# One fused kernel of attention, expert layer and rational layer, all three stages written anew

## What is computed

```python
# attention: B, H, S, D = 2, 8, 768, 64; block 32, window 16
k_sum = k.reshape(B, H, nb, block, D).max(axis=3)
v_sum = v.reshape(B, H, nb, block, D).mean(axis=3)
scores_l = scale * np.matmul(q, k.transpose(0, 1, 3, 2))      # |i - j| < window only
scores_s = scale * np.einsum('bhsd,bhnd->bhsn', q, k_sum) + np.log(block)
a = softmax(concat(masked scores_l, scores_s)); out = a @ concat(v, v_sum)
# expert layer: 1536 tokens x 512, 8 experts of 512 x 1024 x 512, one expert for each token
logits = xn @ en.T / tau; expert_idx = np.argmax(logits, axis=1)
out[mask] = gate_w[mask, None] * (np.maximum(x[mask] @ w1[e], 0.0) @ w2[e])
# rational layer: 512 -> 2048 -> 512
h = x @ w_in; P = a[0] + a[1]*h + a[2]*h*h + a[3]*h*h*h
Q = 1.0 + abs(b[0]) * abs(h) + abs(b[1]) * h*h
out = (P / (Q + 1e-06)) @ w_out
```

## Time and profile before

| | |
|---|---|
| runs | 886.36, 894.67, 916.50 us; median 894.67 |
| profiled execution: span from first to last instruction | 909.4 us |
| instructions | 13113 |
| PE busy, PEld busy | 776.2 us (85%), 641.1 us (71%) |
| DVE, ACT, POOL busy | 505.2, 410.6, 92.5 us |
| mean granted TensorE clock | 0.860 |
| DMA | 80.45 MB, 66388 packets, 43568 of them under 512 B |

### The profile page before, as it was taken

How to read it: one execution, slowest core, us unless ns; L and a number is a source line. 1 busy time by engine, 2 the same in 40 slices (tenths; PEclk the granted TensorE clock), 3 DMA queues, 4 the chain that set the end, 5 groups by cost and what they waited for, 6 DMA issues and landing times.

```text
span 909.4 us, 13113 instructions
## 1 busy us (share of the span) xinstructions
PE 776.2 (85%) x3557; PEld 641.1 (71%) x3558; DVE 505.2 (56%) x911; ACT 410.6 (45%) x752; POOL 92.5 (10%) x107
## 2 busy tenths in 40 slices
PE   2369999999992198887998998849999989999995
PEld 2268989999992176666876876727778768787884
DVE  4822333335455044655333133148999899989996
ACT  2122222234442153655334244146666666666663
POOL 1120302111002300000000000050000000000000
PEclk9655555569995599999999999968999999999999
DMA  9332131133230454787126125030000100000001
GB/s 209 125 107 58 43 99 43 51 95 92 79 107 35 173 210 172 280 279 271 46 92 254 46 74 180 24 92 12 25 21 3 47 0 0 0 25 22 1 0 47
DMA packets 66388, 80.45 MB, mean 88 GB/s; under 512 B 43568, under 2 KB 43568, under 8 KB 65464
## 3 DMA queue, kind: packets, MB, share of 16 engines
q1 hardware_dynamic: 57224, 54.39, 19.5%
q0 software_dynamic: 6048, 20.45, 6.6%
q10 hardware_dynamic: 3088, 5.26, 1.6%
HBM read 63.48 MB, written 16.61 MB: 88 GB/s over the span
## 4 chain that ended last, share of the span: by engine, by line
PE 54%; DVE 18%; DMA 9%; ACT 8%; issue 5%; SPq 3%; POOL 1%; ACTq 0%; DVEq 0%; POOLq 0%
PE bank L1122 12%; PE bank L949 8%; DMA xg<-x_by_slot 7%; PE bank L1101 6%; PE bank L1009 5%; PE bank L1034 5%; PE bank L1175 5%; PE bank L1190 5%; PE bank L1032 4%; PE bank L1007 3%; DVE qd L905 3%; DVE pb L907 3%; DVE rr L906 3%; ACT rr L604 2%; DVE qd L898 2%
## 5 line engine op out<-in xcount | busy, mean ns | idle before, releaser
L1190 PE MATMUL bank<-weights,G 128*128 128x512 f32 x576 | 144.4, 400 | 6.1 <-DVE G L830 5.9
L1175 PE MATMUL bank<-X2T,weights 128*128 (+1 forms) x576 | 145.8, 403 | 1.6 <-DVE X2T L830 1.6
L1190 PEld LDWEIGHTS bank<-weights,G 128*128 128x128 f32 x576 | 108.9, 190 | 34.2 <-DVE G L830 5.8
L1175 PEld LDWEIGHTS bank<-X2T,weights 128*128 128x128 f32 x576 | 109.9, 192 | 28.6 <-issue 2.4
L1101 PE MATMUL bank<-weights,XT 128*128 (+1 forms) x456 | 116.8, 406 | 5.7 <-DVE XT L830 5.7
L1122 PE MATMUL bank<-weights,HT 128*128 x456 | 118.6, 419 | 2.4 <-DVE HT L830 2.4
L488 ACT ACTIVATE es<-es,nmx 128x182 f32<-128x182 f32 x96 | 42.8, 446 | 146.6 <-DVE nmx L736 146.5
L1122 PEld LDWEIGHTS bank<-weights,HT 128*128 128x128 f32 x456 | 90.0, 200 | 23.9 <-issue 2.6
L1101 PEld LDWEIGHTS bank<-weights,XT 128*128 128x128 f32 x456 | 85.2, 191 | 28.2 <-issue 9.6
L736 DVE CUSTOM_DVE_ANT_0 es<-bank,mask_now 128x182 f32<-128x182 f32 x96 | 33.2, 348 | 127.5 <-PE bank L1009 109.7
L830 DVE TENSOR_TENSOR HT<-bank,HT 128x512 fp32r<-128x512 f32 x38 | 24.5, 686 | 97.3 <-ACT HT L549 97.3
(11 more groups left out here) (167 smaller groups left out, 1188.3 us busy)
## 6 DMA issues: line engine op xcount, KB each, us to landing
raw_early<-in_moe_w_dram SPq DMA_DIRECT2D x14, 1024.0 KB, 5.4
raw_late<-in_moe_w_dram SPq DMA_DIRECT2D x14, 1024.0 KB, 8.8
x_by_slot<-x_all ACTq DMA_DIRECT2D x5, 1024.0 KB, 4.4
xg<-x_by_slot POOLq DMA_DIRECT2D x19, 256.0 KB, 5.5
y_by_slot<-yo POOLq DMA_DIRECT2D x19, 256.0 KB, 2.4
raw_early<-in_moe_w_dram POOLq DMA_DIRECT2D x4, 1024.0 KB, 8.4
kraw<-in_k_dram SPq DMA_DIRECT2D x16, 192.0 KB, 4.5
vraw<-in_v_dram SPq DMA_DIRECT2D x3, 1024.0 KB, 6.8
```

Source lines behind the costliest of these rows:

```text
L1175: last = T_.matmul(bank[6 + f % 2][:, :], W[:, 0, wa, kc * F2 + f * P:kc * F2 + (f + 1) * P], X2T[:, bass.ds(c % 2, 1), xa, kc * C_TOK:(kc ...
L1190: last = T_.matmul(bank[tt][:, :], G[:, f % 2, ga, tt * P:(tt + 1) * P], W[:, 1, wa, f * DM:(f + 1) * DM], start=(f == 0 and n_ == 0), sto ...
```

## The change

The same result is computed with the same 19 expert tiles and 48 units, in other steps. Where an order fence stands below, a row is line, operation, what is written, what is read and the shape.

**Set-up.** Keys are loaded as blocks of 32 tokens, 8 KB in a row (3 DMAs of 1 MB). ACT and DVE split them into halves `KHL`, and one PE transpose turns both halves of a token's 64 numbers into a column of 128 (`KTc`). PE sums values for the means with an identity. Zeros for the rows that the first four expert tiles can hold are written to `x_by_slot` here.

**Attention.** There is no loop: 48 units `u` of two heads are written out. POOL splits queries (`split_q`) and copies each tile's keys into `KW` (`windows`); SP swaps the halves of `KW` into `KWs` by four DMAs a tile. A head's scores are two float32r matmuls of 182 columns (`KW`, `KWs`) with one stationary `QS`. `products` takes both heads at once with the values stationary, so x comes out transposed (`OT`), is turned back (`rows_of_x`) and feeds the logits directly. The expert, rank and slot of each tile are worked out while later tiles run, and POOL scatters a tile as soon as its slots are known. POOL also splits expert 0.

The diff, cut to its core:

```diff
-            sp.dma_start(kraw[:, :, h * D:(h + 1) * D], k_src[b, :, h]).then_inc(k_in[b], 16)
+        sp.dma_start(kraw[:, g, :], k_rows[g * P:(g + 1) * P, :]).then_inc(k_in[g], 16)
...
+    def swap_windows(T, half):
+        r, h0 = T % 2, 4 * half
+        sp.wait_ge(kw_done, 2 * T + half + 1)
+        sp.dma_start(KWs[0:D, r, h0:h0 + 4, :].bitcast(F32), KW[D:P, r, h0:h0 + 4, :].bitcast(F32)).then_inc(kws_in[r][half], 16)
+        sp.dma_start(KWs[D:P, r, h0:h0 + 4, :].bitcast(F32), KW[0:D, r, h0:h0 + 4, :].bitcast(F32)).then_inc(kws_in[r][half], 16)
...
+    for e in range(CLEARED):
+        tiles = CLEARED - e
+        sp.dma_start(xs[e * REGION:e * REGION + tiles * P, :].rearrange("(t p) d -> p t d", p=P),
+                     x_all[:, ZERO, :].unsqueeze(1).to_broadcast([P, tiles, DM])).then_inc(cleared_first, 16)
...
+        G_.tensor_copy(qhl[:, r, :, 0, :], heads(qraw[:, r, :])).then_inc(pool_chain, 1)
+        n[0] += 1
+        pool.wait_ge(pool_chain, n[0])
+        G_.tensor_tensor(qhl[:, r, :, 1, :], heads(qraw[:, r, :]), qhl[:, r, :, 0, :].bitcast(F32),
+                         ALU.subtract).then_inc(q_split, 1)
...
+        if T >= 2:
+            pool.wait_ge(s_mm, (T - 2) * H + h0 + 4)
+        bh = b * H + h0
+        at = EDGE + bh * S + t * P - HALO
+        G_.tensor_copy(KW[:, r, h0:h0 + 4, 0:NSUM],
+                       KSs[:, bh * NSUM:(bh + 4) * NSUM].rearrange("c (h n) -> c h n", h=4))
+        G_.tensor_copy(KW[:, r, h0:h0 + 4, NSUM:KEYS],
+                       KTc[:, at:at + 4 * S].rearrange("c (h n) -> c h n", h=4)[:, :, 0:LOC])\
+          .then_inc(kw_done, 1)
...
-    def load_x(i):
-        pool.dma_start(xg[:, :], xs[bass.ds(i * P, P), :]).then_inc(xg_in, 16)
+        row = pool.value_load(row_of[0:1, i:i + 1], min_val=0, max_val=(E - 1) * REGION + N - P)
+        if i >= AHEAD:
+            pool.wait_ge(bx_mm, i - AHEAD + 1)
+        pool.dma_start(xg[i % AHEAD], xs[bass.ds(row, P), :]).then_inc(xg_in[i % AHEAD], 16)
...
-    for T in range(NT):
-        G_.indirect_dma_start(out=xs, out_offset=bass.IndirectOffsetOnAxis(ap=slot_id[:, T:T + 1], axis=0),
-                              in_=x_all[:, T, :], in_offset=None).then_inc(scattered, 16)
-    pool.wait_ge(scattered, 16 * NT)
+        pool.wait_ge(slot_ready, T + 1)
+        pool.wait_ge(x_done, T + 1)
+        if T == 0:
+            pool.wait_ge(cleared_first, 16 * CLEARED)
+        if T == NT - 2:
+            pool.wait_ge(x0_in, 16)
+        G_.indirect_dma_start(out=xs, out_offset=bass.IndirectOffsetOnAxis(ap=slot_id[:, T:T + 1], axis=0),
+                              in_=x_all[:, T, :], in_offset=None).then_inc(scattered, 16)
...
+        slot = (2 * u + i) % 6
+        dve.wait_ge(s_mm, 2 * u + 2)
+        V.tensor_tensor_reduce(
+            es[:, u % 3, i * KEYS:(i + 1) * KEYS], bank[u % 2][:, i * 2 * P:i * 2 * P + KEYS], mask[:, variant(T % TB), :],
+            -SCALE, 3e38, ALU.add, ALU.min, nmx[:, slot:slot + 1]).then_inc(s_read, 1)
...
+        link(V.tensor_reduce(top1[:, T:T + 1], LG[:, T, :], AX.X, ALU.max))
+        link(V.scalar_tensor_tensor(pick[:, r, :], LG[:, T, :], top1[:, T:T + 1], b_[:, IOTA:IOTA + E],
+                                    ALU.is_equal, ALU.mult))
+        link(V.tensor_reduce(first[:, T:T + 1], pick[:, r, :], AX.X, ALU.min))
+        iota = b_[:, IOTA:IOTA + E]
+        V.tensor_tensor(oh[:, T, :], iota, first[:, T:T + 1].to_broadcast([P, E]), ALU.is_equal)\
+         .then_inc(oh_ready, 1)
+                dve.wait_ge(rank_mm, T)
+            V.scalar_tensor_tensor(seen[:, (T + 1) % 2, :], iota, first[:, T:T + 1], seen[:, T % 2, :],
+                                   ALU.is_equal, ALU.add).then_inc(seen_ready, 1)
+        link(V.tensor_tensor(pick[:, r, :], bank[rank_bank(T)][:, H * E:(H + 1) * E], oh[:, T, :], ALU.mult))
+        V.tensor_reduce(slot_id[:, T:T + 1], pick[:, r, :], AX.X, ALU.add).then_inc(slot_ready, 1)
...
-            T_.matmul(S_[:, 0:NSUM], QZ[:, r, h, :],
-                      KS[:, bass.ds(bp, 1), :].rearrange("p s n -> p (s n)"), start=True, stop=True)
-            T_.matmul(S_[:, NSUM:KEYS], QZ[:, r, h, :],
-                      KT[:, bass.ds(bp, 1), bass.ds((j * 2 + r) * P, LOC)]
-                      .rearrange("p s n -> p (s n)"), start=True, stop=True).then_inc(s_mm, 1)
+            pe.wait_ge(s_read, 2 * u - 2)
+        for i in range(2):
+            for keys in (KW, KWs):
+                last = T_.matmul(bank[u % 2][:, i * 2 * P:i * 2 * P + KEYS], QS[:, u // 2 % 2, 2 * (u % 2) + i, :],
+                                 keys[:, r, 2 * p + i, :], start=(keys is KW), stop=(keys is KWs))
+            last.then_inc(s_mm, 1)
...
-            T_.matmul(O_, PT[:, g % 2, i * P:(i + 1) * P], VA[:, r, h * D:(h + 1) * D],
-                      start=True, stop=False)
-            last = T_.matmul(O_, PT[0:KB, g % 2, (2 + i) * P:(3 + i) * P],
-                             VB[0:KB, r, h * D:(h + 1) * D], start=False, stop=True)
+        T_.matmul(O_, VA[:, r, p * P:(p + 1) * P], PT[:, u % 2, 0:2 * P], start=True, stop=False)
+        T_.matmul(O_, VB[0:KB, r, p * P:(p + 1) * P], PT[0:KB, u % 2, 2 * P:4 * P], start=False, stop=True)\
+          .then_inc(pv_mm, 1)
...
+                last = transpose(bank[i % 6][:, r * P:(r + 1) * P],
+                                 KHL[:, g % 2, r0 + r, :, :].rearrange("p a d -> p (a d)").bitcast(F32))
+            last.then_inc(kt_mm, 1)
...
+    def first_rows(T):
+        pe.wait_ge(sel_ready, T - NT + 3)
+        pe.wait_ge(x_done, T + 1)
+        for kc in range(KC):
+            last = T_.matmul(bank[4][:, kc * P:(kc + 1) * P], x_all[:, T, kc * P:(kc + 1) * P], Sel[:, T % 2, :],
+                             start=(T == NT - 2 and kc == 0), stop=(T == NT - 1 and kc == KC - 1))
+        return last
+    def stored_rows():
+        pe.wait_ge(x0_in, 16)
+        for kc in range(KC):
+            T_.matmul(bank[4][:, kc * P:(kc + 1) * P], xg[0][:, kc * P:(kc + 1) * P], ident[:, :],
+                      start=False, stop=False)
+    first_rows(NT - 2)
+    ranks(NT - 1)
+    stored_rows()
+    first_rows(NT - 1).then_inc(bx_mm, 1)
...
-    pe.wait_ge(tab_ready, 1)
-    x_transposes(0)
-    pe.wait_ge(w0_ready, CHUNKS)
-    pe.wait_ge(bx_lo, 1)
-    g1(0, 0, 0)
-    g1(0, 0, 1)
-    x_transposes(1)
-    with pe.Fori(0, MAXT - TAIL) as i:
-        tile_b(i, 2)
+    pe.wait_ge(w0_ready, 2 * CHUNKS)
+    pe.wait_ge(x_done, NT)
+    for k in range(WARM):
+        T_.matmul(bank[6][:, :], W[:, 0, HI, 0:P], W[:, 0, HI, BANK:2 * BANK], start=True, stop=True)
+    pe.wait_ge(bx_lo, 1)
+    g1(0, 0, 0)
+    g1(0, 0, 1)
+    h_transposes(0)
+    g2(0, 0, 0, (0, FC // 2))
+    x_transposes(1)
+    g2(0, 0, 0, (FC // 2, FC))
+    pe.wait_ge(tab_ready, 1)
+    e1, par1 = expert_at(1)
+    pe.wait_ge(half_ready[0], e1 * PER + PER)
+    pe.wait_ge(bx_lo, 2)
+    g1(1, par1, 0)
+    g1(1, par1, 1)
+    x_transposes(2)
+    for i in range(1, MAXT):
+        tile_b(i, min(2, MAXT - 1 - i))
...
+        if i == MAXT - 2:
+            for tt in range(CT):
+                x2_transposes(0, tt)
+        if ahead == 0:
+            c1(0)
+            c1(1)
+        g2(i, par, e)
...
-        A_.activation(qd[:, s, :], h, ACT.Abs, scale=coef[:, 4:5])
-        A_.activation(sq[:, s, :], h, ACT.Square).then_inc(sq_done, 1)
-        A_.activation(pb[:, s, :], h, ACT.Identity, bias=coef[:, 2:3], scale=coef[:, 3:4])
-        A_.activation(pc[:, s, :], h, ACT.Identity, bias=coef[:, 0:1], scale=coef[:, 1:2]).then_inc(h_read, 1)
+        A_.activation(qd[:, s, :], h, ACT.Abs, scale=coef[:, 4:5])
+        A_.activation(sq[:, s, :], h, ACT.Square).then_inc(sq_done, 1)
+        if c > 0 and f == 1:
+            acc_out(c - 1, 1)
+        if u > 0:
+            g_high(u - 1)
+        if c > 0 and f == 1:
+            acc_out(c - 1, 3)
+        A_.activation(pb[s], h, ACT.Identity, bias=ncoef[:, 2:3], scale=ncoef[:, 3:4]).then_inc(lin_done, 1)
...
-        step(1, V.tensor_tensor(g_, g_, h2, ALU.mult))
-        step(2, V.tensor_tensor(g_, g_, p0, ALU.add))
-        dve.wait_ge(r_done, u + 1)
-        step(3, V.scalar_tensor_tensor(q_, q_, 1.0 + 1e-6, r_, ALU.add, ALU.mult))
-        step(4, V.scalar_tensor_tensor(r_, q_, 2.0, r_, ALU.subtract, ALU.mult))
-        step(5, V.scalar_tensor_tensor(g_, g_, -1.0, r_, ALU.mult, ALU.mult))
-        dve.wait_ge(c2_mm, u + 1)
-        V.tensor_copy(G[:, s, HI, :], g_).then_inc(g_hi, 1)
-        dve.wait_ge(g_hi, u + 1)
-        lo_of(G[:, s, LO, :], g_, G[:, s, HI, :]).then_inc(g_done, 1)
+        dve.wait_ge(lin_done, u + 1)
+        step(1, V.tensor_tensor(g_, h, g_, ALU.mult))
+        V.scalar_tensor_tensor(g_, g_, ncoef[:, 1:2], h, ALU.add, ALU.mult).then_inc(h_read, 1)
+        dve.wait_ge(r_done, u + 1)
+        step(2, V.scalar_tensor_tensor(q_, q_, 1.0 + 1e-6, r_, ALU.add, ALU.mult))
+        step(3, V.scalar_tensor_tensor(r_, q_, 2.0, r_, ALU.subtract, ALU.mult))
+        dve.wait_ge(h_read, u + 3)
```

(6 more changed lines are left out.)

1796 lines of the change are left out of this document (1142 added, 654 removed).

## The result

The changed kernel takes 710.98 us (median of four runs, 709.73 to 719.47) against 905.59 us (four runs, 886.36 to 925.37): a ratio of 0.800 with a 95% interval of 0.788 to 0.813. The forecast was 720 us. The profiled execution took 711.2 us, with a span of 709.7.

The account below looks back on a forecast made before the run. PE was taken as the bound, by instruction cost in three stages and by emptiness between them; 909.4 - 20 - 78 - 28 - 32 - 31 = 720 us, range 700 to 792 us.

Parts of the forecast that it names:

- Full clock: Attention: PE likely granted full clock, because new products are wider; at half clock a tile's PE time is about 19 us.
- Attention: Twelve tiles at 11.4 us, of which PE 9.8: 137 us against 215, gain 78.
- the sixth laid on for waits between four busy engines: Attention: 11.4 us a tile, a sixth over PE's 9.8, since four engines at 8 to 10 us have waits.
- Rival one: Attention: PE at half clock, 811 us if in all twelve tiles, 777 at the old share; chance 0.22.
- rival two: Attention: short float32r score matmuls cost more than one pass, 749 us in the middle, 785 at the end; chance 0.15.
- Rival three: Attention: DVE and POOL take turns, 792 us if all steps excluded each other; chance 0.07.
- rivals four and five: Whole kernel: code arrives late, 912 us, chance 0.01; stages don't overlap, waiting for a DMA, 750 us, chance 0.05.
- Set-up: Products start at 41 us instead of 60.8, behind key loads, casts, copies, `KW`, swap and means; gain 20 (4 to 25).
- Experts: 19 tiles at 12.56 us with no wait, plus a surcharge: 248 us against 280.2, gain 32 (20 to 39).
- the surcharge of 7 + 2 us on 19 tiles: Experts: 7 us for a first tile without a neighbour's work and 2 for the rest, on 19 x 12.56.
- Hand-over: Between attention and first `g1`, a chain with logits at half clock: 12 us against 40.0, gain 28 (22 to 31).
- Rational layer: Units at 5.59 us with no wait and no gap ahead: 277 us against 308.0, gain 31 (25 to 36).

Follow-up runs that it names:

- e2: Changed kernel with each attention product of 256 columns cut into four pieces of 64 columns, the stationary operand loaded again for each; 934.07 us.
- e11: Changed kernel with each attention product of 256 columns cut into two pieces of 128 columns; 731.89 us.
- e1: Changed kernel with the attention's score matmuls in full float32 instead of float32r; 745.28 us.
- e3: Changed kernel with one more DVE copy of 182 columns from SBUF to SBUF in each pair of heads, result unused; 723.26 us.
- e8: Changed kernel with the second chunk's key columns copied by ACT ahead of the third chunk's casts; 703.78 us.
- e12: Changed kernel without the four unused matmuls of 512 columns ahead of the first `g1`; 705.33 us.
- e7: Changed kernel with the second half of expert 1's weights split earlier and expert 2's second half loaded ahead of expert 3's first; 706.63 us.
- e5: Changed kernel with weight loads of experts 2 to 7 moving half of the bytes, so results are not the reference's; 705.32 us.
- e4: Changed kernel with two buffers instead of three for the expert stage's tiles of x; 759.71 us.
- e9: Changed kernel with the edits of e7 and e8 together; 700.96 us, ratio 0.790 to the kernel before.
- e10: e9 with the third chunk's key maxima spread over four pairs of heads and its value sums moved later on POOL; 696.99 us, ratio 0.785.

## Why the prediction was right, and where it was not

The terms, against the span of 909.4 us. The two `c1` in the last tile (5.6 us) count for the rational layer, as in the forecast.

| term | forecast | measured | gain forecast | gain measured |
|---|---|---|---|---|
| set-up, products start | 41 | 44.2 | 20 | 16.6 |
| attention | 137 | 125.4 | 78 | 89.6 |
| hand-over | 12 | 7.0 | 28 | 33.0 |
| experts | 248 | 262.2 - 5.6 = 256.6 | 32 | 23.6 |
| rational layer | 277 | 267.9 + 5.6 = 273.5 | 31 | 34.5 |
| tail | 5.4 | 3.0 | 0 | 2.4 |
| sum | 720 | 709.7 | 189 | 199.7 |

The total was right and most of the mechanism with it, but that 720 came so near is luck in part. Set-up and experts are 11.8 us short and the attention 11.6 us too long, which cancels; hand-over, rational layer and tail are 10.9 too long.

- **Full clock**, called the weakest step, held: 1.00 in the attention. The reason given, that the new products are wider, is borne out in part. With pieces of 64 columns the same program has 0.51 (e2); with 128 or 256 it has 0.98 from 60 us on (e11) and 1.00. But width is not all: the kernel before, with 64 columns, had 0.97 for 79.8 us, and in e11 the clock fell for 17 us at the start. Of the 89.6 us gained, cheaper instructions at full clock are 12 x 13.3 - 125.4 = 34 by estimate; the other 55 are the clock.
- **Attention**, the term that was sized worst, with two errors against each other. Products cost 1.15 us, not 0.94, so PE has 10.7 us a tile, not 9.8; but the sixth laid on for waits between four busy engines isn't there. PE idled for 2.6 us in 125, and e1 shows the bound directly: 0.81 us more on PE in each pair lengthened each by 0.78. The other engines had more slack than written down: POOL, DVE and ACT were busy for 87.4, 86.3 and 74.7 us, which is 7.3, 7.2 and 6.2 a tile and not 8.1, 8.4 and 8.4. Rival one falls by the granted clock of 1.00, rival two by the 0.11 us of a score matmul; had the short float32r run like float32, it would have been 38 us by e1, against the 29 to 65 written down. Rival three falls by the length of DVE's steps (0.34 us for 182 columns from PSUM, as before), and e3 shows on which form it would have held. Of rivals four and five nothing shows: PE idled for 2.6 us in the attention and 1.9 in the rational layer, and the hand-over took 7.0.
- **Set-up**, 3.2 us short. The path of the prediction had ACT's copies on it but not the order in which ACT took them: casts of a chunk that landed at 20 us stood ahead of copies that PE waited for. e8 puts it right and gives 38.3, below the forecast. The sum itself doesn't hold either: its terms add up to 40, not 41, and two thirds of 14.5 us of copies are 9.7, not 6. The keys landed at 20.1 us instead of 25, and what follows took 24.1 us where 15 were written down. Of the 5 us for `KW`, swap and means, POOL alone took 5.5 (30.0 to 35.5); scores then started at 39.2, as the prediction says, but products only 5.0 us later.
- **Experts**, 8.6 us short. The step that failed is the surcharge of 7 + 2 us on 19 tiles, which measured 18.5 (256.6 - 19 x 12.53). PE idled for 11.6 us up to 307 (130.4 - 118.8) and had a lowered clock behind waits (0.83 from 190 to 210 us). Of the 18.5 us 2.5 to 4.7 are this execution's own, since six others with the same stage (e1, e2, e3, e8, e11, e12) took 257.5 to 259.7. e7 puts 4 to 6 us down to the order of the first splits and loads; e5 clears the weight stream, although the prediction's "4 MB for each expert of two tiles" was wrong too (in 176 to 307 us the stage carried 254 GB/s, not 160). The third `xg` buffer, costed at part of 32 us, is worth 49.7 by e4.
- **Hand-over**, 5 us better: all of it ran at full clock, where the logits were costed at half; the eleven microseconds of the chain as written down were cut by work that overlapped (x, ranks and selecting records of the last tile lie between 171.1 and 175.2 us).
- **Rational layer**: units at 5.54 instead of 5.59, and of the 5 us for splits and chunk ends PE's waits show 1.8. DVE was busy for 5.0 us a unit (237.8 / 48), near the 4.9 written down, though the steps taken away there would give 4.3 (5.4 - 0.69 - 0.43).

What stays open: the 1.5 us in which ACT stood at 201.4 us for nothing that the trace names (it explains a part of the 3.5 us wait of this execution only), and what lets the clock fall behind one wait and not behind another of the same length, at times at the same place of the same program.

## What to carry to other kernels

Where one engine is busy from end to end, cost its list alone and trust it; give the other engines their slack by measuring, not by a surcharge. Before a rewrite is credited with cheaper instructions, look at the granted clock on both sides: here it was worth more than they were in the attention, and cutting the same products into narrow pieces lost more than the whole change had gained (934.07 us). After such a rewrite the next microseconds lie in the order of two or three list entries at the seams. Moving a handful of them gave 696.99 us against 710.98: 4 to 7 us in the set-up (products from 38.6 instead of 42.9 to 45.8) and 5 to 7 in the experts (252.6 instead of 257.5 to 259.7). The rest lies between executions.

## What the runs showed of the hardware

- PE without a gap is not PE at full clock: 350 us of unbroken work at a mean of 0.51 (e2), in which the pieces had 64 columns.
- A wait of 1.5 us in the attention was followed by about 10 us at half clock (e7); one of 1.56 us in the hand-over was followed by none (e12). One and the same wait in the first attention tile left the clock at 1.00 in one execution (2.21 us, changed kernel) and was followed by a fall to 0.50 in another (2.32 us, e12). The executions of the kernel before that ran beside e9 and e10 lie between 882.93 us at a mean clock of 0.894 and 943.13 us at 0.825, so its scatter goes with the clock too.
- A float32r matmul of 182 columns takes 0.11 us from start to start, in float32 0.31; a float32 product of 64, 128 and 256 columns (two records) takes, where its stationary operand changes each time, 0.36, 0.42 and 0.53 to 0.62 us at full clock (e2, e11, changed kernel), and 0.62 for 64 columns at half clock. So 128 columns cost little more than 64, and 256 a quarter to a half more than 128.
- Nearly all of DVE's copies from SBUF to SBUF that began while POOL computed ended with that instruction or one directly behind it (up to 1.83 us for 0.24 of work); those that lay wholly inside an instruction with which POOL only issues an indirect DMA kept 0.24 to 0.25 (e3).
